# Where a kernel cuts its weights: the low parts of a next matrix in one run, the last refill in halves, the first chunk's operands in halves

## The reference, cut to what matters

```python
x = attention(q, k, v, centroids)          # 2 x 8 heads of 768 x 64, masked by cluster, float32
# a mixture of 8 experts: each of 1536 tokens goes to one
for e in range(8):
    mask = expert_idx == e
    h = np.maximum(x[mask] @ w1[e], 0.0)   # 512 -> 1024
    out[mask] = gate_w[mask, None] * (h @ w2[e])   # 1024 -> 512
# a dense layer over all tokens
h = x @ w_in                               # 512 -> 2048
P = a[0] + a[1]*h + a[2]*h*h + a[3]*h*h*h
Q = 1.0 + abs(b[0])*abs(h) + abs(b[1])*h*h
return (P / (Q + 1e-6)) @ w_out            # 2048 -> 512
```

## Time and profile before

| | us |
|---|---|
| runs of the kernel before | 836.58, 837.04, 841.04 (median 837.04) |
| the profiled execution | 836.16 |
| its span (first to last instruction in the trace) | 834.3 |
| PE busy | 763.8 (92% of the span) |
| DVE busy | 611.2 (73%) |
| ACT busy | 458.1 (55%) |
| POOL busy | 357.4 (43%) |

### The profile page before, as it was taken

One profiled execution on the slowest core, in us unless ns is written; L12 is line 12 of the kernel. 1 busy time (PEld: TensorE's weight loads), 2 busy tenths in 40 slices (PEclk: granted clock), 3 DMA queues, 4 the chain that ended last, 5 costly groups with the idle time before them and its releaser, 6 DMA issues.

```text
span 834.3 us, 15672 instructions
## 1 busy us (share of the span) xinstructions
PE 763.8 (92%) x5407; PEld 715.3 (86%) x5408; DVE 611.2 (73%) x984; ACT 458.1 (55%) x865; POOL 357.4 (43%) x337
## 2 busy tenths in 40 slices
PE   3999999999999892299999999988999999999996
PEld 2899899989998882299999999987999999999995
DVE  2688888888888847156666667679987777778773
ACT  3677777777777752011111111137786776766762
POOL 5566757765665003604333355543232232313232
PEclk9999999999999996599999999999999999999999
DMA  8321111111200016416655456650000000000000
GB/s 243 81 49 29 39 28 47 28 38 28 48 35 1 0 50 220 136 27 227 210 191 169 160 179 223 201 202 1 1 13 14 1 26 1 26 0 25 0 26 25
DMA packets 67907, 63.59 MB, mean 76 GB/s; under 512 B 30872, under 2 KB 53528, under 8 KB 67872
## 3 DMA queue, kind: packets, MB, share of 16 engines
q1 hardware_dynamic: 65952, 56.85, 21.7%
q0 software_dynamic: 1920, 6.30, 2.0%
HBM read 56.32 MB, written 6.82 MB: 76 GB/s over the span
## 4 chain that ended last, share of the span: by engine, by line
PE 50%; issue 24%; DVE 13%; POOL 8%; ACT 3%; DMA 1%; POOLq 0%; DVEq 0%; SPq 0%; ACTq 0%
PE PS L502 8%; PE PS L503 8%; PE PS L504 8%; PE PS L381 7%; POOL HL L872 5%; PE PS L356 3%; PE PS L357 3%; PE PS L341 3%; PE PS L342 3%; PE PS L323 3%; DVE NM L924 2%; DVE PTL L985 1%; DVE w_low L969 1%; POOL out L881 1%; PE PS L365 1%
## 5 line engine op out<-in xcount | busy, mean ns | idle before, releaser
L502 PE MATMUL PS<-XH,w_high 128*128 128x256 f32 x640 | 183.2, 286 | 7.7 <-DVE XL L1149 3.6
L503 PE MATMUL PS<-XL,w_high 128*128 128x256 f32 x640 | 182.8, 286 | 0.0
L504 PE MATMUL PS<-XH,w_low 128*128 128x256 f32 x640 | 182.6, 285 | 0.0
L801 POOL TENSOR_SCALAR w_high<-w_raw 128x1024 fp32r<-128x1024 f32 x80 | 101.4, 1287 | 131.6 <-DMA w_raw<-in_moe_w 107.4
L872 POOL TENSOR_TENSOR HL<-U,HH 128x512 fp32r<-128x512 f32 x48 | 62.6, 1303 | 184.5 <-ACT HH L741 184.5
L502 PEld LDWEIGHTS PS<-XH,w_high 128*128 128x128 f32 x640 | 124.5, 195 | 10.6 <-issue 8.8
L985 DVE TENSOR_TENSOR PTL<-PS,PTH 128x384 fp32r<-128x384 f32 x192 | 98.5, 552 | 40.7 <-ACT PTH L650 40.7
L503 PEld LDWEIGHTS PS<-XL,w_high 128*128 128x128 f32 x640 | 124.5, 194 | 1.8
L504 PEld LDWEIGHTS PS<-XH,w_low 128*128 128x128 f32 x640 | 124.4, 194 | 0.0
L969 DVE TENSOR_TENSOR w_low<-w_raw,w_high 128x1024 fp32r<-128x1024 f32 x80 | 114.6, 1459 | 9.2 <-issue 9.2
L650 ACT ACTIVATE PTH<-PS 128x384 fp32r<-128x384 f32 x192 | 84.8, 489 | 47.0 <-PE PS L381 46.0
(11 more groups left out here) (171 smaller groups left out, 1726.6 us busy)
## 6 DMA issues: line engine op xcount, KB each, us to landing
w_raw<-in_moe_w SPq DMA_DIRECT2D x64, 512.0 KB, 7.9
xs<-xs_dram SPq DMA_DIRECT2D x9, 513.0 KB, 3.8
w_raw<-in_moe_w_in SPq DMA_DIRECT2D x8, 512.0 KB, 8.3
w_raw<-in_moe_w_out SPq DMA_DIRECT2D x8, 512.0 KB, 7.9
QK<-in_q SPq DMA_DIRECT2D x16, 192.0 KB, 3.1
QK<-in_k SPq DMA_DIRECT2D x16, 192.0 KB, 3.3
V<-in_v SPq DMA_DIRECT2D x16, 192.0 KB, 2.4
xs_dram<-zeros SPq DMA_DIRECT2D x1, 513.0 KB, 3.9
```

Of the source, the lines that this page charges most:

```text
L502: nc.tensor.matmul(o, wh, xh, start=first, stop=False)
L503: nc.tensor.matmul(o, wh, xl, start=False, stop=False)
L504: return nc.tensor.matmul(o, wl, xh, start=False, stop=last)
L801: return nc.gpsimd.tensor_scalar(HIGH[par][:, p, :], RAW[par][:, p, :], 1.0, 0.0, ALU.mult, ALU.add)
```

## The change

It has four parts.

1. DVE's `chunk` makes all eight low pieces of matrix e + 1 in one run after `XL` of the next chunk, ahead of the copy into `YT`. The pieces 4 to 7 of matrix e, which stood between the `HL` of expert e, are gone from there. Low pieces 4 to 7 of matrix 0 move ahead of the first `cut_chunk(0)`; those of `w_in`, which stood ahead of the layer's first step, are now made in expert 7.
2. SP loads the first four pieces of `w_out` once the four banks of expert 7's first product are done (`h_ps`), and the other four after `used_up(E - 1)`.
3. `cut_results` works in two halves of the features in all chunks: two ACT and two DVE instructions of 512 numbers for one of 1024 each. The wait on `y_dve` stands before ACT's second half in chunk 0.
4. PE waits for one half (feature tiles 0 and 1) before its first matmul of a chunk and for the other before tile 2. Its waits on `y_act` and `y_dve` ahead of the layer are gone.

```diff
@@ SP
             load_columns(0, w_in, range(8))
+            total, = bounds(sp, E - 1, (1,))
+            sp.wait_ge(h_ps, 4 * total)
+            load_rows(1, w_out, range(4), 0)
             used_up(E - 1)
-            load_rows(1, w_out, range(8), 0)
+            load_rows(1, w_out, range(4, 8), 0)
@@ PE
-            def hidden(o, piece, par, xpar):
+            def hidden(o, piece, par, xpar, halves=None):
                 for f in range(2):
                     for c in range(KD):
+                        if halves is not None and f == 0 and c % 2 == 0:
+                            pe.wait_ge(yl_done, halves + c // 2 + 1)
...
-                if j == 0:
-                    pe.wait_ge(yl_done, c + 1)
...
-                hidden(PS[:, j % 4, :], j, 0, cpar).then_inc(g3_done, 1)
+                hidden(PS[:, j % 4, :], j, 0, cpar, 2 * c if j == 0 else None).then_inc(g3_done, 1)
...
-            total, = bounds(pe, E - 1, (1,))
-            pe.wait_ge(y_act, total + 1)
-            pe.wait_ge(y_dve, total + 1)
             layer_chunk(0, 0, start=True)
@@ ACT
-                nc.scalar.activation(XH[cpar][:, :, :], YT[:, :, bass.ds(c * CH, CH)], ACT.Copy).then_inc(yh_done, 1)
+                for n in range(2):
+                    part = slice(2 * n, 2 * n + 2)
+                    if n and isinstance(c, int) and c == 0:
+                        act.wait_ge(y_dve, bounds(act, E - 1, (1,))[0] + 1)
+                    nc.scalar.activation(XH[cpar][:, part, :], YT[:, part, bass.ds(c * CH, CH)], ACT.Copy).then_inc(yh_done, 1)
...
             act.wait_ge(y_act, total + 1)
-            act.wait_ge(y_dve, total + 1)
             act.wait_ge(xl_done, total + 1)
@@ DVE
             def chunk(i, lo, off, e=None, par=0):
                 for fp in range(4):
-                    if e is not None:
-                        low_piece(e, par, 4 + fp)
                     dve.wait_ge(hh_done, 4 * i + fp + 1)
...
                 cut_chunk(i + 1)
                 if e is not None:
-                    for p in range(4):
+                    for p in range(8):
                         low_piece(e + 1, 1 - par, p)
                 dve.wait_ge(y_ps, 2 * i + 2)
...
             dve.drain().then_inc(y_dve, 1)
+            for p in range(4, 8):
+                low_piece(0, 0, p)
             cut_chunk(0)
...
             def cut_results(c, cpar):
-                dve.wait_ge(yh_done, c + 1)
-                nc.vector.tensor_tensor(XL[cpar][:, :, :], YT[:, :, bass.ds(c * CH, CH)], XH[cpar][:, :, :].bitcast(F32),
-                                        ALU.subtract).then_inc(yl_done, 1)
+                for n in range(2):
+                    part = slice(2 * n, 2 * n + 2)
+                    dve.wait_ge(yh_done, 2 * c + n + 1)
+                    nc.vector.tensor_tensor(XL[cpar][:, part, :], YT[:, part, bass.ds(c * CH, CH)], XH[cpar][:, part, :].bitcast(F32),
+                                            ALU.subtract).then_inc(yl_done, 1)
...
             cut_results(0, 0)
-            for p in range(4, 8):
-                low_piece(E, 0, p)
             layer_chunk(0, 0, start=True)
```

## The result

The changed kernel takes 840.64 us (median of 22 runs, 838.74 to 844.94), the kernel before, in as many runs beside it, 838.40 (835.64 to 841.04). The ratio is 1.0031 with a 95% interval of 1.0017 to 1.0044: 1.4 to 3.7 us slower, a change of less than the 0.5% (4.2 us) that bounded the forecast. The forecast was +0.5 us, 837.5 us in all, with 835.5 to 839.5 as its own band and 833.5 to 841 for 8 in 10. The median of 840.64 lies outside that band and inside the wider one; of the 3.1 us that it is above 837.5, 1.36 are in the kernel before as well (838.40 against the 837.04 that the forecast started from). The profiled execution took 840.41 us.

The account below looks back on a forecast made before the run. PE was taken to bound the kernel, with only the seam's 9.1 us of gaps and half-clock slumps to win. +2.15 and -1.65 gave +0.5 us, a median of 837.5 us; range 833.5 to 841 for 8 in 10.

Parts of the forecast that it names:

- DVE's run in expert 7: Expert 7's eight low pieces beside POOL's: run near 14 us, copy into `YT` at 552.3, 4.5 us late.
- The price of a POOL piece: In expert 7, each POOL `w_high` piece beside DVE's low pieces lengthens DVE's run by 0.68 to 0.85 us.
- The halves: At the seam, 2.0 us from the copy's start to PE in place of 3.34; PE starts 3.1 us later.
- The slump after the seam: PE at half clock after idling 6.8 us: 2.25 us lost in place of 1.55, bounds 1.55 and 3.4.
- The way to the second product: Layer's first chunk: 9.28 us from ACT to PE, not 10.86; PE at 568.7, +2.15 us; gap 2.3 to 0.6.
- I let the second slump go: -1.65: Layer's first chunk: no half clock after the shrunken gap before the second product, 1.65 us won.
- a wait of PE would make it wrong: Sign against the prediction: PE waiting anywhere within an expert, or in chunks 1 to 5.
- The low pieces at the router: Matrix 0's pieces 4 to 7 on DVE beside POOL's scatter: cost 0, bound four issues at +0.3, +1.3 us.
- Rival C: At the router, the scatter is slowed: +1.3 us on top of the forecast, 838.8 us; chance 0.05.
- Low runs in experts 0 to 6: All eight low pieces in one run before the copy into `YT` cost PE nothing: price 0, bound 0.
- Rival A: Expert 7: the refill doesn't disturb DVE, copy at 549.2, second slump gone; -3.2 us, 833.8 us; chance 0.15.
- Rival B: End of expert 7: the late copy outweighs everything, second slump stays; +3.05 us, 840.1 us; chance 0.20.

Follow-up runs that it names:

- no_early_refill: The changed kernel without part 2: all eight pieces of `w_out` asked for after expert 7's second product; ratio to the kernel before 1.0004.
- halves_alone: The kernel before with parts 3 and 4 alone, `XH` and `XL` made in halves; ratio to the kernel before 0.9993.
- router_back: The changed kernel with low pieces 4 to 7 of matrix 0 put back behind the first `cut_chunk(0)`; ratio to the kernel before 1.0013.
- wout_in_idle: The changed kernel with low pieces 0 to 3 of `w_out` made ahead of the layer's first step, in DVE's idle time; ratio to the kernel before 0.9993.
- scatter_beside_sbuf: The kernel before with eight unused DVE instructions added beside the scatter, both inputs in SBUF; one profile, not timed.
- scatter_beside_psum: The kernel before with eight unused DVE instructions added beside the scatter, one input in PSUM; one profile, not timed.
- best_of_both: As five_in_the_run, with low pieces 0 and 1 of `w_out` made ahead of the layer's first step; ratio to the kernel before 0.9980.
- refill_and_halves: The kernel before with parts 2, 3 and 4 and not part 1; ratio to the kernel before 0.9974.
- five_in_the_run: As refill_and_halves, with five low pieces of the next matrix in place of four in each expert's run; ratio to the kernel before 0.9967.

## Why the prediction was right or wrong

- *DVE's run in expert 7* was right: forecast about 14 us and a copy 4.5 us late, measured 14.24 and 4.6 (4.88 less 0.30). The price of a POOL piece, forecast at 0.68 to 0.85 us, was 0.83 over all six and 0.88 by no_early_refill.
- *The halves*: 2.0 us from the copy to PE forecast, 1.67 measured; the gap 6.8 forecast, 6.55 measured. Right.
- *The slump after the seam*: 2.25 us taken; ACT's first result came 4.68 us behind PE's start, 3.15 is that distance at full clock (halves_alone), so 1.5 was lost. Too high here, but router_back lost 2.4 behind the same gap. The slumps before were also a little oversized: matmuls stand 0.213 us apart at half clock and 0.12 at full, so that 3.1 and 3.3 us at half clock lose about 1.4 us each and not 1.55 and 1.65.
- *The way to the second product*: 568.7 forecast, 2.15 us late; measured 1.6 late behind expert 7's end. The 0.6 us of gap was 0.78. Right.
- *"I let the second slump go: -1.65"*. The slump did go, and the term was wrong all the same. This step failed: it took PE's own lost time for the bound. From D on, DVE's chain was. The 1.65 us came back as 1.66 us of waiting for `OUT`, in chunk 1, where the prediction said that a wait of PE would make it wrong. In PE's own terms: the gap grew by 2.9 us, the slump behind it by 0.15, the wait for `HL` fell by 1.5 and the second slump's 1.4 went, +0.2 in all; the wait for `OUT` added 1.66 less the 0.23 that were there before, and that is the 1.6 us of C. The term could have been questioned ahead of the result: the chain of the kernel before runs along DVE. In DVE's terms, D came 3.06 us later and the chain got 1.44 shorter, +1.62. Of the 1.44, the prediction had only the 0.35 at the instruction at 562.24, and not the low piece of step 1 beside POOL, of which no row was shown: 2.35 us then, 1.22 now. The test of it is wout_in_idle, which left PE's start alone and took 2.9 us from C at the same D.
- *The low pieces at the router, "I take 0"*: wrong. About +1.3 us, by coincidence the bound given (two issues at +1.0 us and not four at +0.3). The row at 669.61 was one instruction of 0.75 us beside the issue and no test of a low piece of 1.2. The rule that seemed to confirm it (the Trainium skill, "SBUF — State Buffer", section "Who interferes with whom": such a `tensor_tensor` takes only the read interface, and descriptor generation needs the write interface, marked there as inferred) is not borne out: 1.99 and 1.97 us in place of 0.96 beside the low pieces, 1.05 to 1.15 beside the shorter instructions of scatter_beside_sbuf, and 0.96 when one input of these is in PSUM. Rival C had 5% and was what happened, beside the forecast's own mechanism; its 838.8, 1.8 us above before, is the nearest of all to the measured 2.2.
- *Low runs in experts 0 to 6, price 0*: right as far as the profiles show, 195.85 against 195.83 us.
- *Rival A* was out: POOL's four pieces did stand beside the run. *Rival B* named the late copy, the right place of the loss; its price came from a second slump that didn't come.

In sum: +1.6 at the seam and +1.3 at the scatter are +2.9, the measured ratio gives +1.4 to +3.7. The forecast of +0.5 was within its range because -1.65 too much and +1.3 too little are small, not because the sum was right: that part is luck.

## What to carry to other kernels

When PE's gap or slump is mended, ask which in-order engine is next late, and look for it in the chain that ended last: a busy PE without waits may still be paced by an engine that will stop it one chunk later. A cover that is moved (weights cut earlier, loads asked for earlier) meets whatever it stands beside at the new place; here the early refill and the long run of low parts cost each other 3.5 us of DVE's time, and once the long run was left out, C became 3.6 us shorter than before in one profile and the time 0.26% less. A row for "not slowed" counts only for an instruction as long as the one that is moved.

## What the runs showed of the hardware

- A DVE `tensor_tensor` with two SBUF inputs can slow POOL's issue of an indirect DMA: 1.99 and 1.97 in place of 0.96 us beside pieces of 1.2 us, 1.05 to 1.15 beside ones of 0.7, not at all with one input in PSUM. Not every issue beside such work is longer: the one at 333.31 kept its 0.96 us, and so did that at 669.61 before.
- When a DVE low piece and POOL's `HL` meet, one of the two takes about 1 us more, and which one it is changed with 0.13 us: 2.35 and 1.27 us when they start together (before), 1.24 and 2.23 when the low piece is ahead by that much (scatter_beside_psum). With an unchanged seam this alone moved C by 0.8 us.
- The same idle time of PE can be followed by half clock or not: after 1.73 us of idling halves_alone went on at full clock (ACT's first result 3.15 us later), best_of_both at half (5.30 us, of which 0.41 is a wait for the second half of `XL`). After 2.14 us refill_and_halves went on at full clock (3.15 us), after 2.45 five_in_the_run at half (4.65). After 6.55 and 6.56 us it was 4.68 and 5.59. This alone moves a profile by 1 to 2 us, as much as most of what was sought here; what sets it stays open.
